# The half-filled last products of v and u moved behind the scores and put side by side in the row halves of the TensorE array

## The chip, the core and the metric

The kernel runs on one core of a Trainium2 chip. Its time is the device time of one execution in microseconds (us). Of the kernel before, three runs took 307.78, 306.66 and 303.63 us, a median of 306.66. A fourth execution was recorded by the hardware profiler and took 303.61 us.

## The reference: what is computed

Three blocks follow each other, for 2 batches of 768 tokens, all in 32-bit floats.

1. A gated recurrent attention (mLSTM) of 8 heads of 40 features. Per step t: C = f C + i v k^T, n = f n + i k, y = sigmoid(o) * (C q) / max(|n q|, 1), with stabilised gates. Its output x has 8 * 40 = 320 features per token.
2. A gated MLP: h = relu(x @ w_in), w_in of 320 x 1024; u is the first half of the 1024 columns, v the second. v is normalised over its 512 columns, mixed over the tokens with w_spatial (768 x 768), a bias is added, the result is multiplied by u and by w_out.
3. A second MLP with a token shift: k = relu(xk @ w_k), out = sigmoid(xr @ w_r) * (k*k @ w_v).

The change touches x @ w_in of block 2 alone.

## The kernel before

**Tiling.** The 1536 tokens are 12 chunks of 128 (NU = 12). The attention works by chunk, in its chunked form: scores of the 128 queries against the 128 keys, values, a carried state between chunks. Products that want more precision than the one-pass type float32r are made of parts: a tensor is split in hi (rounded) and lo (the rest), and hi*hi + hi*lo + lo*hi is summed in PSUM.

**x @ w_in.** x has 320 features, so its feature-major copy is three tiles of 128, 128 and 64 rows: TA, TB and TL ("left"). The TL tile has its 64 features twice, in the rows 0 to 63 and 64 to 127 of the array; xth holds the hi parts and xtl the lo parts, each twice. Tile 4 of win holds the hi part of the last 64 rows of w_in in the rows 0 to 63 and their lo part in the rows 64 to 127. `parts` (L1265) so makes eight products: three for TA, three for TB, and two for TL. The first TL product (win tile 4 by xth) gives hi*hi + lo*hi, all 128 rows put to use. The second (win tile 4 by xtl) gives hi*lo, which is wanted, and lo*lo, which isn't: it is the half-filled product. `v_product(u)` (L1376) has x as the stationary operand and moves 512 columns of w_in, into bank ps_v, for one chunk. `u_product(g, m)` (L1400) has 128 columns of w_in as the stationary operand and moves 384 tokens (three chunks, a block g) of x, into bank ps_e. Both call `chain` (L1251), whose matmul is L1254.

**Order of the work.** All of it is written out by hand, an engine's program each, tied by semaphores. TensorE's runs over slots u = 2 to 13. A slot holds, in this order: `state(u-1)` (L1358, bank ps_z), `values(u-1, 1)` (L1339, ps_in), `carry(u-1)` (L1349, ps_out), `scores(u)` (L1329, ps_s0 and ps_s1), `v_product(u-2)`, in slots 3 and 4 `spread_decay(u)` (L1294), up to slot 4 `factors_to_tokens(u+1)` (L1283), `values(u, 0)`, one `u_product`, `x_transposed(u-1)` (L1368, ps_t), and in slots 7, 10 and 13 a second `u_product`. The u products lie in slots 4 to 13 (`u_tiles`), as x of a block of three chunks must be there. Scores are 64-row products: heads of the one group lie in the rows 0 to 63 of the array, of the other in 64 to 127, and the two alternate, into two banks.

**The other engines.** ScalarE reads ps_v (L644) and ps_e (`u_relu`, L661), rounds x (L655) and the parts of w_in (`win_left_hi`, L681 and L682), and takes the exponentials (L637). The hi of the last 64 rows that is subtracted for lo lies for a while in a free place of vnh (`win_left`). VectorE multiplies scores by exponentials (L946), makes x from values and gates (L980 to L1008, `outputs`), takes lo of x (L1026) and of w_in (`win_lo_of`, L1050), adds the state (L972), copies decays (L938) and normalises v. GpSimd and the DMA queues play no part in the change. After slot 13 TensorE runs the groups of blocks 2 and 3, one after the other (all L1254), with the eight banks in turn.

Of the kernel before, what the change touches and what calls it, by code (L numbers as in the profile page):

```python
# [27 lines left out]
ACT = mybir.ActivationFunctionType  # L28

B, H, S, D = 2, 8, 768, 40  # L30
DM, DF = H * D, 1024
HF = DF // 2
CH = 128
NC = S // CH
NU = B * NC
# [6 lines left out]
NB = 384  # L42
NBLK = B * S // NB
UPB = NB // CH
# [3 lines left out]
TA, TB, TL = 0, 1, 2  # L48
# [35 lines left out]
def u_tiles(slot):  # L84

    out = []
    for g in range(NU // UPB):
        first = UPB * g + UPB + 1
        for m, s in enumerate((first, first + 1, first + 2, first + 3)):
            if s == slot and g < NU // UPB - 1:  # L90
                out.append((g, m))
    return out
# [3 lines left out]
U_AT = {x: n for n, x in enumerate(U_ORDER)}  # L96
# [98 lines left out]
def program(nc, qk, vk, og, fg, ig, w_in, w_sp, b_sp, mu, w_out, w_k, w_v, w_r, out):  # L195
# [14 lines left out]
    win = at("win", [128, 5, DF], WIN, F32R)  # L210
    win_raw = at("win_raw", [128, 3, DF], WIN + 8192)
    ut = at("ut", [128, B, 4, S], UT)
    vnh = [at(f"vnh{b}", [128, NC, HF], VN + b * 24576, F32R) for b in range(B)]
# [10 lines left out]
    xtl = at("xtl", [128, 2, 3, NB], XT + 9216, F32R)  # L224
# [96 lines left out]
    with ExitStack() as ctx:  # L321
        names = ["ps_s0", "ps_s1", "ps_e", "ps_in", "ps_out", "ps_z", "ps_t", "ps_v"]
        ps_s0, ps_s1, ps_e, ps_in, ps_out, ps_z, ps_t, ps_v = [
            ctx.enter_context(nc.psum_tensor(n, [128, 512], F32)) for n in names]
# [15 lines left out]
        sems = {}  # L340
# [12 lines left out]
        def win_left(n):  # L353

            if n == 0:
                return vnh[0][64:128, NC - 2, :]
            return vnh[0][64:128, NC - 1, 128 * (n - 1):128 * n]

        def bits(ap):

            return ap.bitcast(F32)
# [232 lines left out]
        def _(act):  # L594
            sc = nc.scalar
# [82 lines left out]
            def win_left_hi(n):  # L678
                c = WIN_PART[n]
                act.wait_ge(sems[f"win_in{min(n, 1)}"], 64)  # L680
                sc.activation(win_left(n), win_raw[64:128, 2, c], ACT.Copy).then_inc(sems["win_left"], 1)  # L681
                sc.activation(win[0:64, 4, c], win_raw[0:64, 2, c], ACT.Copy).then_inc(sems["win_hi"], 1)  # L682

            def win_rows_hi(n):
                c = WIN_PART[n]
# [122 lines left out]
            for p, key in enumerate(GROUPS):  # L808
# [36 lines left out]
                if kind == "k":  # L845
                    n = 8 * a + b
# [28 lines left out]
        def _(dve):  # L875
            ve = nc.vector
# [170 lines left out]
            def win_lo_of(n):  # L1047
                c = WIN_PART[n]
                dve.wait_ge(sems["win_left"], n + 1)
                ve.tensor_tensor(win[64:128, 4, c], win_raw[64:128, 2, c], bits(win_left(n)),  # L1050
                                 ALU.subtract).then_inc(sems["win_left_lo"], 1)
                dve.wait_ge(sems["win_hi"], 3 * n + 3)
                ve.tensor_tensor(win[:, 2, c], win_raw[:, 0, c], bits(win[:, 0, c]),
                                 ALU.subtract).then_inc(sems["win_lo"], 1)
# [122 lines left out]
            for p, key in enumerate(GROUPS):  # L1177
                kind, a, b = key
                ps = bank_of[p % 8]
                if kind == "sp":  # L1180
                    n = 4 * a + b
# [41 lines left out]
                if kind == "k":  # L1223
                    n = 8 * a + b
# [12 lines left out]
                if kind == "v":  # L1237
                    n = UPB * a + b
# [9 lines left out]
        def _(pe):  # L1248
            te = nc.tensor

            def chain(dst, pairs):  # L1251

                for n, (w, x) in enumerate(pairs):
                    last = te.matmul(dst, w, x, start=n == 0, stop=n == len(pairs) - 1)  # L1254
                return last

            def parts(w, x):

                out = []
                for t in (TA, TB):
                    out += [(w(0, t), x(0, t)), (w(0, t), x(1, t)), (w(1, t), x(0, t))]
                return out + [(w(0, TL), x(0, TL)), (w(1, TL), x(1, TL))]  # L1265

            def split_rows(w, cols):

                def tile(part, t):
                    return w[:, 4 if t == TL else t + 2 * part, cols]  # L1270
                return tile
# [99 lines left out]
            def x_tiles(g, cols):  # L1371
                def tile(part, t):
                    return (xth, xtl)[part][:, g % 2, t, cols]
                return tile

            def v_product(u):  # L1376
                pe.wait_ge(sems["xt_hi_done"], u + 1)
                pe.wait_ge(sems["xt_lo_done"], u + 1)
                if u == 0:

                    pe.wait_ge(sems["win_hi"], 3)
                    pe.wait_ge(sems["win_left_lo"], 1)
                    pe.wait_ge(sems["win_lo"], 1)
                    pe.wait_ge(sems["win_lo_pool"], 1)
                if u == 0:
                    pe.wait_ge(sems["exp_done"], 2 * EARLY)
                pe.wait_ge(sems["v_read"], u)
                x = x_tiles(u // UPB, slice((u % UPB) * CH, (u % UPB + 1) * CH))
                chain(ps_v[:, :], [(x_, w_) for w_, x_ in parts(split_rows(win, slice(HF, DF)), x)]
                      ).then_inc(sems["v_mm"], 1)  # L1390

            def u_chain(dst, g, m):
                if g == 0:
                    pe.wait_ge(sems["win_hi"], 3 * (m + 2))
                    pe.wait_ge(sems["win_left_lo"], m + 2)
                    pe.wait_ge(sems["win_lo"], m + 2)
                    pe.wait_ge(sems["win_lo_pool"], m + 2)
                return chain(dst, parts(split_rows(win, slice(m * 128, m * 128 + 128)), x_tiles(g, slice(0, NB))))

            def u_product(g, m):  # L1400
                pe.wait_ge(sems["gwt_done"], 5)
                pe.wait_ge(sems["u_read"], U_AT[g, m])
                u_chain(ps_e[:, 0:NB], g, m).then_inc(sems["u_mm"], 1)


            pe.wait_ge(sems["vr_zero"], 1)
# [18 lines left out]
            for u in range(2, NU + 2):  # L1425
                if u == 2:
                    spread_decay(2)
                if u <= NU:
                    if chunk(u - 1) < NC - 1:
                        state(u - 1)  # L1430
                    if u == 4:
                        x_transposed(2)
                    values(u - 1, 1)
                    if chunk(u - 1) > 0:
                        carry(u - 1)
                    if u in (2, 3):
                        x_transposed(u - 2)
                if u < NU:
                    scores(u)
                if u == NU + 1:  # L1440

                    u_product(*u_tiles(u)[0])
                v_product(u - 2)
                if 3 <= u < NC - 1:
                    spread_decay(u)
                if u < NC - 1:
                    factors_to_tokens(u + 1)
                if u < NU:
                    values(u, 0)
                if u_tiles(u) and u <= NU:  # L1450
                    u_product(*u_tiles(u)[0])
                if 4 <= u <= NU:
                    x_transposed(u - 1)
                for g, m in u_tiles(u)[1:]:
                    u_product(g, m)
# [3 lines left out]
            for p, key in enumerate(GROUPS):  # L1459
# [4 lines left out]
                if kind == "u":  # L1464
                    last = u_chain(ps[:, 0:NB], a, b)
                elif kind == "sp":
# [12 lines left out]
                    pairs = []  # L1479
# [111 lines left out]
```

## Time and profile before

| what | us |
|---|---|
| three runs | 307.78, 306.66, 303.63 |
| the profiled execution's own time | 303.61 |
| its span, first to last instruction | 301.9 |
| TensorE matmuls busy in it | 291.7 (97%) |
| VectorE busy | 203.1 (67%) |
| ScalarE busy | 160.6 (53%) |
| GpSimd busy | 65.0 (22%) |
| mean granted clock of TensorE | 0.983 of full |

The own time is 1.7 us above the span. In the rows below PE is TensorE, PEld its weight loads, DVE VectorE, ACT ScalarE. A matmul of 32-bit floats is two records, one of float32r is one. Matmuls are pipelined, so a record's length is mostly latency, and what a product costs is read from start to start.

### The profile page before, as it was taken

How to read it: one execution, taken by the hardware profiler on the slowest of the kernel's cores; microseconds unless marked ns; L12 is line 12 of the kernel's file. 1: busy time of each engine (PE TensorE's matmuls, PEld its weight loads, DVE VectorE, ACT ScalarE, POOL GpSimd, SP SyncE). 2: the span in 40 equal slices, each digit the busy share in tenths (PEclk: the TensorE clock that was granted, in tenths of full speed). 3: DMA queues.
4: the chain of work that ended last, by engine and by line, in shares of the span. 5: the costliest groups of instructions: out<-in, count | busy, mean ns of one | idle time of the engine just before them, and what ended most of it. 6: DMA issues, size and time to landing. Idle time of an engine off the chain costs nothing.

```text
span 301.9 us, 5393 instructions
## 1 busy us (share of the span) xinstructions
PE 291.7 (97%) x1904; PEld 278.6 (92%) x1904; DVE 203.1 (67%) x434; ACT 160.6 (53%) x365; POOL 65.0 (22%) x93
## 2 busy tenths in 40 slices
PE   7999898999999999999999999998999999999996
PEld 3898787998999898999999999997999999999995
DVE  6899889898788588446416888768764276655111
ACT  5747675793456456331136567598672467255000
POOL 6143345343344332612101203200000000000000
PEclk9977979999999999999999999999999999999999
DMA  4779951473472162000060020500001000100111
GB/s 133 229 212 280 334 163 66 157 213 105 138 245 85 21 244 88 0 2 0 14 196 0 0 67 1 175 2 0 0 2 43 22 2 2 46 22 0 43 46 43
DMA packets 12922, 25.99 MB, mean 86 GB/s; under 512 B 2016, under 2 KB 5696, under 8 KB 12896
## 3 DMA queue, kind: packets, MB, share of 16 engines
q1 hardware_dynamic: 12720, 25.12, 27.2%
q10 hardware_dynamic: 176, 0.53, 0.4%
q8 instruction: 15, 0.25, 0.3%
q14 instruction: 11, 0.09, 0.1%
HBM read 23.63 MB, written 2.02 MB: 85 GB/s over the span
## 4 chain that ended last, share of the span: by engine, by line
PE 88%; DVE 5%; ACT 3%; DMA 2%; issue 1%; SPq 0%; ACTq 0%; DVEq 0%
PE ps_v L1254 15%; PE ps_e L1254 13%; PE ps_s L1254 12%; PE ps_out L1254 7%; PE ps_in L1254 7%; PE ps_t L1254 7%; PE ps_in L1339 6%; PE ps_z L1254 6%; PE ps_s L1329 5%; PE ps_out L1349 3%; DMA wv_raw<-in_w_v 2%; PE ps_z L1358 2%; PE ps_v L1408 2%; PE ps_t L1368 1%; DVE pt L946 1%
## 5 line engine op out<-in xcount | busy, mean ns | idle before, releaser
L1339 PEld LDWEIGHTS ps_in<-tok,pt 128*128 128x128 f32 x192 | 24.6, 197 | 2.0 <-DVE pt L946 1.3
L1226 DVE TENSOR_TENSOR kr<-kr 128x384 f32<-128x384 f32 x32 | 17.7, 558 | 12.5 <-ACT kr L850 12.5
L1339 PE MATMUL ps_in<-tok,pt 128*128 128x42 f32 x192 | 25.1, 282 | 0.7 <-DVE pt L946 0.7
L637 ACT ACTIVATE et<-mb,gwt 128x128 f32<-128x128 f32 x80 | 24.7, 392 | 1.0 <-POOL mb L546 0.9
L822 ACT ACTIVATE gh<-ut 128x384 fp32r<-128x384 f32 x16 | 8.4, 525 | 30.2 <-DVE ut L1192 30.2
L1254 PE MATMUL ps_v<-win,xth 128*128 128x512 f32 x60 | 21.5, 423 | 0.1
L585 POOL TENSOR_TENSOR gl<-ut,gh 128x384 fp32r<-128x384 f32 x8 | 9.0, 1122 | 53.1 <-ACT gh L822 53.1
L1254 PE MATMUL ps_e<-xth,win 128*128 128x384 f32 x60 | 17.3, 353 | 0.9 <-ACT ut L661 0.9
L1174 DVE TENSOR_TENSOR kkl<-kr,kkh 128x384 fp32r<-128x384 f32 x32 | 17.7, 553 | 0.7
L946 DVE TENSOR_TENSOR pt<-ps_s,et 128x512 f32<-128x512 f32 x24 | 16.5, 688 | 1.4 <-PE ps_s L1329 0.7
L806 ACT ACTIVATE kkh<-kr 128x384 fp32r<-128x384 f32 x32 | 16.7, 522 | 1.3 <-DVE kr L1226 1.3
L1165 DVE SCALAR_TENSOR_TENSOR shifted<-yt,omm,scaled 128x384 f32<-128x384 f32 x24 | 15.3, 641 | 2.6 <-ACT scaled L801 2.0
L539 POOL TENSOR_SCALAR rstd<-mv 128x1 f32<-128x1 f32 x12 | 6.1, 508 | 45.8 <-DVE mv L1014 45.8
L1329 PE MATMUL ps_s<-qkt 64*128 64x128 f32 x192 | 15.8, 310 | 0.0
L648 ACT ACTIVATE vnh<-vnf 128x512 fp32r<-128x512 f32 x12 | 7.6, 634 | 14.4 <-DVE vnf L1019 14.3
L1254 PEld LDWEIGHTS ps_v<-win,xth 128*128 128x128 f32 x60 | 11.6, 194 | 3.8 <-issue 0.7
L801 ACT ACTIVATE scaled<-yt,mucol 128x384 f32<-128x384 f32 x24 | 14.6, 606 | 0.1
L1329 PEld LDWEIGHTS ps_s<-qkt 64*128 64x128 f32 x192 | 13.3, 210 | 1.3 <-issue 0.7
L1254 PE MATMUL ps_v<-win,xtl 128*128 128x512 f32 x36 | 14.3, 398 | 0.0
L661 ACT ACTIVATE ut<-ps_e 128x384 f32<-128x384 f32 x12 | 5.9, 490 | 13.1 <-PE ps_e L1254 13.1
L1254 PEld LDWEIGHTS ps_e<-xth,win 128*128 128x128 f32 x60 | 11.0, 188 | 1.7 <-issue 1.6
L1349 PE MATMUL ps_out<-zt,qkt 128*128 128x84 f32 x80 | 12.2, 301 | 0.0
(325 smaller groups left out, 883.1 us busy)
## 6 DMA issues: line engine op xcount, KB each, us to landing
mb<-maxima SPq DMA_DIRECT2D x9, 512.0 KB, 5.8
tok<-in_vk SPq DMA_DIRECT2D x12, 328.0 KB, 4.3
qkt<-in_qk SPq DMA_DIRECT2D x24, 160.0 KB
sp_raw<-in_w_sp SPq DMA_DIRECT2D x6, 384.0 KB, 5.0
out_y<-ob SPq DMA_DIRECT2D x12, 160.0 KB, 1.8
wv_raw<-in_w_v SPq DMA_DIRECT2D x2, 640.0 KB, 5.3
win_raw<-in_w_in SPq DMA_DIRECT2D x4, 256.0 KB, 6.1
wk_raw<-in_w_k SPq DMA_DIRECT2D x2, 512.0 KB, 4.7
```

Source lines behind the costliest of these rows:

```text
L585: gp.tensor_tensor(g[1][:, b, :], ut[:, a // 2, b, (a % 2) * NB:(a % 2) * NB + NB], bits(g[0][:, b, :]), ALU.subtract).then_inc(sems["g_lo ...
L637: last = sc.activation(et[:, j, h, :], mb[u % 2][:, HH * j + h, :], ACT.Exp, bias=gwt[:, chunk(u), x:x + 1], scale=-1.0)
L801: sc.activation(scaled[:, n % 2, :], yt[a % 2][:, t, 1:NB + 1], ACT.Copy, scale=mucol[:, w, t:t + 1]).then_inc(sems["x_scaled"], 1)
L806: sc.activation(kkh[(n // 8) % 2][:, n % 8, :], kr[n % 4][:, :], ACT.Copy).then_inc(sems["kk_hi_done"], 1)
L946: ve.tensor_tensor(pt[:, j, :, :], ps_s[j][:, :].rearrange("p (h t) -> p h t", h=HH), et[:, j, :, :], ALU.mult).then_inc(sems["probs_done" ...
L1165: ve.scalar_tensor_tensor(shifted[:, n % 2, :], y[:, t, 0:NB], omm[:, w, t:t + 1], scaled[:, n % 2, :], ALU.mult, ALU.add).then_inc(sems[" ...
L1174: ve.tensor_tensor(kkl[(n // 8) % 2][:, n % 8, :], kr[n % 4][:, :], bits(kkh[(n // 8) % 2][:, n % 8, :]), ALU.subtract).then_inc(sems["kk_ ...
L1226: ve.tensor_tensor(kr[n % 4][:, :], kr[n % 4][:, :], kr[n % 4][:, :], ALU.mult).then_inc(sems["kk_done"], 1)
L1254: last = te.matmul(dst, w, x, start=n == 0, stop=n == len(pairs) - 1)
L1329: last = te.matmul(ps_s[r][:, g * CH:(g + 1) * CH], keys[u % NS][rows, g, :], queries[u % NS][rows, g, :], start=True, stop=True)
L1339: last = te.matmul(p_in[:, HH * j + h, :], pt[:, j, h, :], vt[u % 2][:, HH * j + h, :], start=True, stop=True)
L1349: last = te.matmul(p_out.rearrange("p (r g) d -> p r g d", r=2)[:, :, g, :], queries[u % NS][:, g, :], zt[(u - 1) % 2][:, g, :, :], start= ...
```

## The change

Tile 4 of win is swapped for the v columns (part 0): hi now lies in the rows 64 to 127 and lo in 0 to 63; the u columns stay as they were. In the slots 4 to 11 a new `left_products` is issued right behind `scores(u)`: it makes only hi*lo of the last 64 features, for v in the array's rows 64 to 127 into ps_v, and for the slot's first u product in the rows 0 to 63 into ps_e. These two open the accumulation in their banks. In the same slots `v_product` and the first `u_product` go on in the open bank, with seven products each and no longer the eighth. The slots 2, 3, 12 and 13, the second u products of the slots 7 and 10, and the u products that follow the slots are as before.

```diff
         def win_left(n):
             if n == 0:
-                return vnh[0][64:128, NC - 2, :]
+                return vnh[0][0:64, NC - 2, :]
             return vnh[0][64:128, NC - 1, 128 * (n - 1):128 * n]
+        def left_rows(n):
+            return (slice(0, 64), slice(64, 128)) if n == 0 else (slice(64, 128), slice(0, 64))
...
-                sc.activation(win_left(n), win_raw[64:128, 2, c], ACT.Copy).then_inc(sems["win_left"], 1)
-                sc.activation(win[0:64, 4, c], win_raw[0:64, 2, c], ACT.Copy).then_inc(sems["win_hi"], 1)
+                lo, hi = left_rows(n)
+                sc.activation(win_left(n), win_raw[lo, 2, c], ACT.Copy).then_inc(sems["win_left"], 1)
+                sc.activation(win[hi, 4, c], win_raw[hi, 2, c], ACT.Copy).then_inc(sems["win_hi"], 1)
...
-                ve.tensor_tensor(win[64:128, 4, c], win_raw[64:128, 2, c], bits(win_left(n)),
+                lo, _ = left_rows(n)
+                ve.tensor_tensor(win[lo, 4, c], win_raw[lo, 2, c], bits(win_left(n)),
...
-            def chain(dst, pairs):
+            def chain(dst, pairs, opened=False):
-                    last = te.matmul(dst, w, x, start=n == 0, stop=n == len(pairs) - 1)
+                    last = te.matmul(dst, w, x, start=n == 0 and not opened, stop=n == len(pairs) - 1)
-            def parts(w, x):
+            def parts(w, x, opened=False):
-                return out + [(w(0, TL), x(0, TL)), (w(1, TL), x(1, TL))]
+                return out + [(w(0, TL), x(0, TL))] + ([] if opened else [(w(1, TL), x(1, TL))])
...
+            def left_products(u, g, m):
+                pe.wait_ge(sems["xt_hi_done"], u + 1)
+                pe.wait_ge(sems["xt_lo_done"], u + 1)
+                pe.wait_ge(sems["v_read"], u)
+                pe.wait_ge(sems["win_hi"], 3 * (m + 1) + 1 if g == 0 else 15)
+                pe.wait_ge(sems["gwt_done"], 5)
+                pe.wait_ge(sems["u_read"], U_AT[g, m])
+                t = slice((u % UPB) * CH, (u % UPB + 1) * CH)
+                te.matmul(ps_v[:, :], xtl[64:128, (u // UPB) % 2, TL, t], win[64:128, 4, HF:DF], start=True, stop=False)
+                te.matmul(ps_e[:, 0:NB], win[0:64, 4, m * 128:m * 128 + 128], xtl[0:64, g % 2, TL, :],
+                          start=True, stop=False)
...
-                v_product(u - 2)
+                opened = u < NU and len(u_tiles(u)) > 0
+                if opened:
+                    left_products(u - 2, *u_tiles(u)[0])
+                v_product(u - 2, opened)
...
                 if u_tiles(u) and u <= NU:
-                    u_product(*u_tiles(u)[0])
+                    u_product(*u_tiles(u)[0], opened)
```

## Rows read from the trace of the kernel before

**Rows 1.** The page's busy shares, and the busy time of three stretches (clock before DMA).
```profile
PE 291.7 (97%) x1904; PEld 278.6 (92%) x1904; DVE 203.1 (67%) x434; ACT 160.6 (53%) x365; POOL 65.0 (22%) x93
...
49.00:111.00 62.00, 61.31 (x487) 56.72 (x485) 51.09 (x127) 37.09 (x98) 25.84 (x36) 1.00 0.45 141
119.90:205.00 85.10, 85.10 (x494) 85.10 (x493) 53.97 (x93) 44.53 (x88) 16.93 (x16) 1.00 0.14 41
207.20:298.90 91.70, 91.70 (x584) 91.62 (x584) 46.89 (x91) 40.50 (x88) 0.00 (x0) 1.00 0.06 21
```
**Rows 2.** TensorE's waits, 49 to 111 us (the slots 5 to 11): total, times, longest.
```profile
PE ps_e L1254 <- ACT ut L661: 0.7, 2, 0.3
```
**Rows 3.** TensorE's timeline in slot 9: start, length, engine, line, operation, count.
```profile
85.12 1.16 PE L1329 MATMUL ps_s<-qkt 64*128 64x128 f32 x16
86.21 0.50 PE L1254 MATMUL ps_v<-win,xth 128*128 128x512 f32 x1
86.55 0.39 PE L1254 MATMUL ps_v<-win,xtl 128*128 128x512 f32 x1
...
88.17 0.98 PE L1339 MATMUL ps_in<-tok,pt 128*128 128x42 f32 x8
88.98 0.42 PE L1254 MATMUL ps_e<-xth,win 128*128 128x384 f32 x1
89.24 0.34 PE L1254 MATMUL ps_e<-xtl,win 128*128 128x384 f32 x1
...
90.47 0.49 PE L1368 MATMUL ps_t<-ident,xg 128*128 128x128 f32 x3
90.80 0.88 PE L1358 MATMUL ps_z<-tok,kw 128*104 128x84 f32 x8
```
**Rows 4.** The last two records of the scores, in flight at 86.19 us; all scores of slots 5 to 11.
```profile
86.00 0.28 PE L1329 MATMUL ps_s<-qkt 64*128 64x128 f32 x2
...
L1329 PE MATMUL ps_s<-qkt x112: 272/272/373, 51.6 to 104.5; 64*128 64x128 f32 x112
```
**Rows 5.** TensorE's timeline in slot 4, and the granted clock (0.50) from 39.64 us.
```profile
40.40 2.08 PE L1329 MATMUL ps_s<-qkt 64*128 64x128 f32 x16
42.41 0.78 PE L1254 MATMUL ps_v<-win,xth 128*128 128x512 f32 x1
...
44.66 0.29 PE L1294 MATMUL ps_z<-gwt,ident 128*128 128x16 f32 x2
...
48.60 0.55 PE L1368 MATMUL ps_t<-ident,xg 128*128 128x128 f32 x3 [1.21 <-DVE xg L1008]
39.64:43.04 3.40, 3.40 (x23) 0.50 0.25 72
```
**Rows 6.** VectorE's timeline in slot 4.
```profile
44.99 0.17 DVE L938 COPY dec<-ps_z 128x16 f32<-128x16 f32 x1 [1.30 <-PE ps_z L1294]
```
**Rows 7.** Before slot 7's and slot 8's v product: lo of x on VectorE; u_relu on ScalarE.
```profile
65.56 0.55 DVE L1026 TENSOR_TENSOR xtl<-ps_t,xth 128x384 fp32r<-128x384 f32 x1
...
67.53 0.50 PE L1254 MATMUL ps_v<-win,xth 128*128 128x512 f32 x1
...
74.45 0.49 ACT L661 ACTIVATE ut<-ps_e 128x384 f32<-128x384 f32 x1 [1.45 <-PE ps_e L1254]
...
77.93 0.50 PE L1254 MATMUL ps_v<-win,xth 128*128 128x512 f32 x1
```
**Rows 8.** Slot 7: the last step of x on VectorE, and what follows on TensorE.
```profile
71.56 0.20 DVE L1008 COPY xg<-xg 128x64 f32<-128x64 f32 x1
...
71.93 0.49 PE L1368 MATMUL ps_t<-ident,xg 128*128 128x128 f32 x3
72.77 0.41 PE L1254 MATMUL ps_e<-xth,win 128*128 128x384 f32 x1 [0.34 <-ACT ut L661]
```
**Rows 9.** The last step of x on VectorE in slot 9; VectorE's waits, 49 to 111 us.
```profile
89.71 0.20 DVE L1008 COPY xg<-xg 128x64 f32<-128x64 f32 x1
...
DVE inter L980 <- PE ps_out L1349: 4.2, 5, 1.1
```

More of the change, by code:

```diff
@@ L1374, in x_tiles, with v_product @@
                 return tile
-            def v_product(u):
+            def v_product(u, opened=False):
                 pe.wait_ge(sems["xt_hi_done"], u + 1)
@@ L1388, in v_product, with u_chain @@
                 x = x_tiles(u // UPB, slice((u % UPB) * CH, (u % UPB + 1) * CH))
-                chain(ps_v[:, :], [(x_, w_) for w_, x_ in parts(split_rows(win, slice(HF, DF)), x)]
-                      ).then_inc(sems["v_mm"], 1)
-            def u_chain(dst, g, m):
+                chain(ps_v[:, :], [(x_, w_) for w_, x_ in parts(split_rows(win, slice(HF, DF)), x, opened)],
+                      opened).then_inc(sems["v_mm"], 1)
+            def left_products(u, g, m):
[9 more added lines that the diff above has]
+                          start=True, stop=False)
+            def u_chain(dst, g, m, opened=False):
                 if g == 0:
@@ L1397, in u_chain, with u_product @@
                     pe.wait_ge(sems["win_lo_pool"], m + 2)
-                return chain(dst, parts(split_rows(win, slice(m * 128, m * 128 + 128)), x_tiles(g, slice(0, NB))))
-            def u_product(g, m):
+                return chain(dst, parts(split_rows(win, slice(m * 128, m * 128 + 128)), x_tiles(g, slice(0, NB)), opened),
+                             opened)
+            def u_product(g, m, opened=False):
                 pe.wait_ge(sems["gwt_done"], 5)
                 pe.wait_ge(sems["u_read"], U_AT[g, m])
-                u_chain(ps_e[:, 0:NB], g, m).then_inc(sems["u_mm"], 1)
+                u_chain(ps_e[:, 0:NB], g, m, opened).then_inc(sems["u_mm"], 1)
             pe.wait_ge(sems["vr_zero"], 1)
```

## The prediction

> **What bounds the kernel now.** I read the page's busy shares first, then the busy time by stretch, then TensorE's waits, and last its timeline slot by slot. TensorE is busy for 97% of the span, and in the stretches that matter it is more than that: from 49 to 111 us, the slots 5 to 11, it lacks 0.7 of 62 us, and in the two long stretches of the MLP groups it lacks nothing [rows 1]. In the slots 5 to 11 its only wait is that of the second u products of the slots 7 and 10 for their bank, 0.7 us in all [rows 2]. So what TensorE is spared in these slots comes off the end, as long as nothing else is late within the same slot. Slot 4 is the exception: its transposes start 1.21 us late, for VectorE's x [rows 5].
>
> **What is taken away.** In each of eight slots one v product of 512 columns and one u product of 384. Their cost is the distance from start to start, not the record's length. In slot 9 the second v product starts at 86.55 and the next work at 88.17: seven products in 1.62 us, 0.23 each. The second u product starts at 89.24 and the transposes at 90.47: seven in 1.23, 0.18 each [rows 3]. The first product of either chain costs more (0.34 and 0.26), but it stays the first. Taken away per slot: 0.23 + 0.18 = 0.41 us.
>
> **What is added.** Two products of 64 rows, one in each row half, 512 and 384 columns. The trace shows no float32r product in a row half, but it shows the scores. In slot 9 their last two records start together, at 86.00, and both are over 0.28 us later, when a single one takes 0.272 [rows 4]. Sixteen records take 1.09 us (85.12 to 86.21), 0.07 each, where full-height transposes with as many columns take 0.11 each (three in 90.47 to 90.80) [rows 3]. So the two halves do run side by side, a pair per 0.11 us. If the new pair does so too, it costs what its longer member costs, 0.23 us. The change of the array from halves to full height is paid now as well: the first v product starts at 86.21, 0.21 us behind the last pair [rows 3, 4], where the next pair would have come after 0.11; the other 0.10 is the change. It is paid once, before and after, as the new pair stands in the same mode as the scores. **Bounds:** from below 0.13, if the pair's stream hid that 0.10; from above, one behind the other, 0.41; and further up, one behind the other at the pace of a 32-bit record of the scores (0.11 us for 128 columns, 0.87 ns a column), 0.45 + 0.34 = 0.79 us. I take 0.23, because the scores are the nearest rows: the same row halves, two banks, straight before. Per slot 0.41 - 0.23 = 0.18 us is saved.
>
> The Trainium skill has a rule that speaks for less: its page "TensorE: Matmul & The Clock Gate", section "Measured speedup vs the span model", gives 3.07 times for four products of 32 rows and 512 columns, not four times. By that shortfall, an estimate, the pair would cost 0.23 * 4 / 3.07 = 0.30 us and a slot would save 0.11. Rows 4 show no such loss for the scores.
>
> **Slot 4.** Here the u product's saving goes into the wait that is there anyway: the transposes wait for VectorE's x, and the chain to it starts with the decays (L938) at 44.99, which wait for the small product at 44.66 behind v [rows 5, 6]. What counts in this slot is thus when v ends. In the profiled execution the granted clock is 0.50 from 39.64 to 43.04 and the scores of this slot take 2.01 us instead of 1.09, 1.84 times as long [rows 3, 5]. The new pair stands at 42.3 in that stretch: 0.23 * 1.84 = 0.43. The v product that is gone stood behind 43.04, at 0.23. So v ends 0.20 later, and so do the decays, x and the slot. In an execution where the clock is full here, it is 0.0.
>
> **The waits that are added** stand in front of v, where v's own already stood: x of the chunk, and ps_v read. Lo of x is there at 66.11 in slot 7 for a v at 67.53, 1.4 us ahead [rows 7], and that is the least of the eight slots. New are the bank of u and its weights. The bank was read last by u_relu of the slot before; the tightest place is slot 8, where u_relu ends at 74.94 and v starts behind the scores at 77.93, 3 us later [rows 7]. In slot 11 it stands alike. The hi part of w_in is made a slot ahead. All this costs nothing. If such a wait did bite, v, the values and the u product would be queued behind it, and VectorE's probabilities would not be, since the scores are already out. The swapped halves of tile 4 are the same number of instructions over as many rows on ScalarE and VectorE: nothing. No DMA is moved, and no queue of SyncE or GpSimd is passed.
>
> **What is late next.** The transposes in each slot now come 0.18 earlier against VectorE's chain. In slot 9 x is ready at 89.91 for a start at 90.47, 0.56 ahead [rows 3, 9], enough. In slot 7 it is ready at 71.76 for 71.93: 0.11 of the 0.18 fits [rows 8] and some 0.06 is lost before the transposes. But behind them the second u product waits for u_relu until 72.77, and that goes by the end of the first u product, so nothing of it reaches the slot's end. The savings of earlier slots move VectorE along with TensorE: it waits for the carried product in five of the slots, 4.2 us in all [rows 9], and has slack to follow. Behind the slots TensorE has no idle time that could swallow anything in the stretches shown [rows 1].
>
> **The sum.** Seven slots at 0.176 (0.231 + 0.176 - 0.231) are 1.23 us off, slot 4 gives 0.20 back: 1.0 us off. The profiled execution, 303.61 us with 301.9 of span and 1.7 around it, becomes 302.6. The runs of before spread over 4 us: two executions at 303.6, two at 306.7 and 307.8, with a mean of the four of 305.4 and a median of the three of 306.66. Less 1.0 these are 304.4 and 305.7. A median of the changed kernel is as likely by the one as by the other, so I say **305.0 us**, which is 1.0 below a base of 306.0.
>
> **The rivals**, on the same base of 306.0 us.
> *Side by side, but not wholly:* the pair costs between 0.23 and 0.41, with the middle, 0.32, as its mark. Then a slot saves 0.09, seven save 0.6, and slot 4 gives back 0.32 * 1.84 - 0.23 = 0.36: 0.3 off, 305.7. For it speaks that the members are of unequal length, which the scores' are not; against it, rows 4. Chance 0.12. By the page's estimate, 0.30, it would be 0.11 a slot, 0.8, less 0.3 in slot 4: 305.5.
> *The change doesn't do what it says:* the halves run one behind the other, at 0.41. The seven slots give nothing, and slot 4 loses 0.41 * 1.84 - 0.23 = 0.5 us: 306.5. For it: nothing shown of float32r in halves. Against it: the scores use the same two row halves and two banks [rows 4]. Chance 0.10.
> *Slower, one mechanism:* a half-height float32r product streams like a record of the scores, at 0.87 ns a column. Its place is the pair in each slot. Side by side it costs 0.45, 0.04 more than was saved: 0.3 for seven slots, and 0.45 * 1.84 - 0.23 = 0.6 in slot 4, 0.9 slower, 306.9. Behind each other it costs 0.79: 7 * 0.38 and 0.79 * 1.84 - 0.23 = 1.2 in slot 4, 3.9 slower, 309.9. It decides from a pair of 0.41 us on. For it: 0.11 us for 128 columns in the scores; against: that is equally the time of a weight load, as the full-height values of 42 columns start no closer (eight in 88.17 to 88.98) [rows 3]. Chance 0.06 and 0.02.
>
> **How the numbers follow.** The forecast, 1.0 off, has 0.70; the rivals have 0.12, 0.10 and 0.08. The range is mostly the spread of the runs: its low end is the fast executions less the full saving with slot 4 at full clock, 303.6 - 1.4 = 302.2; its high end is the slow ones, 307.3 as a mean, less 0.1, which takes in the first two rivals: 307.2. About 2 in 10 are left out. What a measurement of this kernel tells from no change is about 2%, 6.1 us. To be faster by that, each of eight slots would have to save 0.77 us, more than the two products cost together: 0.01. To be slower by it the pair would have to cost 1.2 us: 0.02. Within 2%: 0.97.
>
> **What would show it.** In the timeline of slot 9 two float32r records of 64 rows should start within 0.01 us of each other, 0.11 behind the last scores; the first full v product should start some 0.44 us behind the last scores, not 0.21; scores to the end of v should stay as long as before, and the u chain should be 0.18 shorter. The scores of the slots 5 to 11, from 51.6 to 104.5 [rows 4], should stand 1.1 us closer together. Two 64-row records with starts 0.2 us apart would show the second rival, a first v product 0.65 behind the scores the third. A wait of TensorE for ut or xtl in front of the pair would prove me wrong on the waits, and a wait for xg in more slots than 4 and 7 would prove me wrong on VectorE's slack.

## The result, and the profile after

The changed kernel took 304.08 us, the median of 20 runs from 299.32 to 308.18, beside 306.19 for the kernel before (20 runs, 302.80 to 309.20). The ratio is 0.990, 95% interval [0.985, 0.994]: 1% faster, within the 2% that counts as the same. In a second series the same kernel came out at 305.39 (12 runs) beside 305.00 (35 runs), ratio 1.008 [1.003, 1.012]. (A ratio leaves out, of either kernel, the executions more than 1.5% above its own fastest, so it can differ from the ratio of the medians, which is 0.993 in the first series and 1.001 in the second.) The two intervals exclude each other, so one ratio alone is not to be trusted here; what the change is worth has to be read from the trace.

The profiled execution took 302.88 us with a span of 301.2. The page's shares and the two long MLP stretches are as before, TensorE without a gap in them [rows 1]; the columns are TensorE, weight loads, VectorE, ScalarE, GpSimd, then clock and DMA:

```profile
PE 290.9 (97%) x1904; PEld 276.5 (92%) x1904; DVE 202.4 (67%) x434; ACT 160.5 (53%) x365; POOL 64.0 (21%) x93
...
49.40:110.50 61.10, 60.34 (x488) 54.98 (x486) 50.93 (x127) 37.04 (x98) 25.53 (x36) 1.00 0.45 143
119.38:204.48 85.10, 85.10 (x494) 85.10 (x493) 53.95 (x93) 44.72 (x88) 16.93 (x16) 1.00 0.13 41
206.70:298.20 91.50, 91.50 (x584) 91.40 (x583) 46.66 (x91) 40.30 (x88) 0.00 (x0) 1.00 0.06 21
```

TensorE's timeline of slot 9 of the changed kernel answers to [rows 3]:

```profile
85.10 1.16 PE L1336 MATMUL ps_s<-qkt 64*128 64x128 f32 x16
86.01 0.42 PE L1409 MATMUL ps_e<-xtl,win 64*128 64x384 f32 x1
86.02 0.48 PE L1408 MATMUL ps_v<-win,xtl 64*128 64x512 f32 x1
86.43 0.50 PE L1261 MATMUL ps_v<-win,xth 128*128 128x512 f32 x1
...
88.16 0.98 PE L1346 MATMUL ps_in<-tok,pt 128*128 128x42 f32 x8
88.97 0.42 PE L1261 MATMUL ps_e<-xth,win 128*128 128x384 f32 x1
...
90.28 0.49 PE L1375 MATMUL ps_t<-ident,xg 128*128 128x128 f32 x3
```

The two new products (L1409 and L1408) start within 0.01 us of each other. From the scores' start to the values it takes 3.06 us, where it took 3.05 before (85.12 to 88.17): the pair costs what v's last product cost. From the u product's start to the transposes it takes 1.31 instead of 1.49: the 0.18 of the u product is gone.

The lengths of the slots, from the first record of the scores to the next slot's (slot 11: to v behind it), read from the traces of the profiled executions, before, after and of the experiments that follow. From slot 5 on, after and again, the one kernel that was profiled twice, agree to 0.01 us; and where two kernels do the same work in a slot other than 7, they agree to 0.02 us, in executions from 299 to 306 us. So the slots tell hundredths where the clocked times don't tell a microsecond:

```
kernel        slot 3   slot 4   slot 5  6     7      8     9     10     11    sum 5 to 11
before          9.02    11.18    7.52  7.34  10.40  8.28  8.27  10.25  7.38   59.44
after           8.69    11.49    7.35  7.17  10.44  8.10  8.10  10.09  7.20   58.45
again          10.23    10.92    7.35  7.17  10.44  8.10  8.10  10.09  7.20   58.45
same_half       9.58    12.37    7.52  7.34  10.27  8.28  8.28  10.27  7.38   59.34
from_slot5     10.06    10.91    7.35  7.17  10.44  8.09  8.10  10.09  7.20   58.44
lo_early       11.27    11.33    7.35  7.32  11.35  8.09  8.10  10.09  7.21   59.51
lo_prev        10.17    11.09    7.35  7.17  10.10  8.10  8.10  10.09  7.20   58.11
short_mask      9.55    11.28    7.34  7.17  10.09  8.11  8.10  10.09  7.20   58.10
v_alone         9.66    12.12    7.53  7.35  10.38  8.27  8.28  10.27  7.39   59.47
den_early       7.93     8.39    7.34  7.17  10.10  8.09  8.10  10.09  7.20   58.09
den_before      7.92     8.55    7.52  7.34  10.26  8.27  8.28  10.25  7.38   59.30
```

Six of the seven slots from 5 on are 0.16 to 0.18 us shorter after the change. Slot 7 is not: it is 0.04 longer.

### The profile page after: what moved, and what is told of

It is laid out like the page before. It is cut to its first block, busy times and chain, and to the rows that moved or that the text cites. A ratio compares the mean times of both kernels' runs of the same rounds, so it can differ in the third digit from the quotient of the medians.

```text
span 301.2 us, 5417 instructions
## 1 busy us (share of the span) xinstructions
PE 290.9 (97%) x1904; PEld 276.5 (92%) x1904; DVE 202.4 (67%) x434; ACT 160.5 (53%) x365; POOL 64.0 (21%) x93
## 4 chain that ended last, share of the span: by engine, by line
PE 90%; DVE 5%; ACT 3%; issue 1%; DVEq 0%; ACTq 0%
PE ps_v L1261 15%; PE ps_s L1261 13%; PE ps_e L1261 13%; PE ps_out L1261 7%; PE ps_t L1261 7%; PE ps_in L1261 7%; PE ps_z L1261 7%; PE ps_in L1346 6%; PE ps_s L1336 5%; PE ps_out L1356 3%; PE ps_z L1365 2%; PE ps_v L1429 2%; PE ps_t L1375 1%; DVE pt L952 1%; DVE den L997 1%
## 5 line engine op out<-in xcount | busy, mean ns | idle before, releaser
L795 ACT ACTIVATE xr<-shifted 128x384 fp32r<-128x384 f32 x12 | 6.3, 522 | 10.9 <-DVE shifted L1172 10.9
```

## The experiments

**again: the changed kernel once more.** No edit.

> The changed kernel once more. Theory A (the profile's sum): it is 0.7 to 1.1 us faster than the kernel before, ratio 0.9965, and what the first comparison showed beyond that (about 1%, 3 us) is the scatter of the granted clock between executions. Theory B: the change saves some 3 us, of which the two profiled executions show only a part; then the ratio is again at 0.99 or below. In the profile the pair's two records start 0.006 us apart and scores to the end of v take 3.05 us as before.

Measured: slots 5 to 11 as after, to 0.01 us; median 305.39, ratio 1.008 [1.003, 1.012]. Theory B is out. The slots bear out theory A, but its ratio of 0.9965 lies outside the interval as well: a ratio of these series is not good to half a per cent. Up to slot 5 the executions differ: slot 3 takes 8.69 us in after and 10.23 in again, slot 4 11.49 and 10.92, with where the stretches of granted clock 0.5 fall and how long they are. In this execution they go from 20.0 to 26.8 and from 40.5 to 43.9; in the others each is 3.4 or 6.8 us long, or the first is absent. Over the kernel before, the changed one and three of its variants (same_half, from_slot5, lo_early), the execution time goes with the mean granted clock, 2.1 us for each 0.01. With that slope taken out, 32 executions of the changed kernel stand 0.9 us below the 63 of the kernel before whose clock was recorded, with a standard error of 0.27. So the gain is 0.4 to 1.4 us (95%), and the traces' 1.0 in the slots 5 to 11 lies in it.

**same_half: both products in the same row half.**

```diff
-            return vnh[0][64:128, NC - 1, 128 * (n - 1):128 * n]
+            return vnh[0][0:64, NC - 1, 128 * (n - 1):128 * n]
-            return (slice(0, 64), slice(64, 128)) if n == 0 else (slice(64, 128), slice(0, 64))
+            return slice(0, 64), slice(64, 128)
...
-                te.matmul(ps_e[:, 0:NB], win[0:64, 4, m * 128:m * 128 + 128], xtl[0:64, g % 2, TL, :],
+                te.matmul(ps_e[:, 0:NB], win[64:128, 4, m * 128:m * 128 + 128], xtl[64:128, g % 2, TL, :],
```

> Changed kernel, but all parts of win's tile 4 are swapped and both new products lie in the rows 64 to 127: same instructions, same place, same waits, only not in different halves. Theory side by side: they now run one behind the other, the pair costs 0.41 us instead of 0.23 (0.60 us from the first to the first full v product instead of 0.41), 0.18 more in each of slots 5, 6, 8 to 11, so 1.1 to 1.3 us slower than the changed kernel. Rival (a half-height product is cheap by itself, or it is only the place behind the scores that helps): no difference to the changed kernel.

TensorE's timeline of slot 9 in same_half:

```profile
87.46 0.48 PE L1408 MATMUL ps_v<-win,xtl 64*128 64x512 f32 x1
87.78 0.33 PE L1409 MATMUL ps_e<-xtl,win 64*128 64x384 f32 x1
88.04 0.50 PE L1261 MATMUL ps_v<-win,xth 128*128 128x512 f32 x1
```

Now the u product starts 0.32 us behind the v product, and the first full product 0.58 behind, where it was 0.41. Slots 5, 6 and 8 to 11 are as long as in the kernel before, to 0.02 us, and together 1.06 us longer than in after; slot 7, at 10.27, is shorter than in both (see lo_prev). The saving is all from lying side by side; a half-height product by itself is not cheaper, and the place behind the scores gives nothing. The times (305.26 median, ratio 1.005 [1.000, 1.010]) agree but would not have shown it.

**v_alone: only v in its half.** The u product of `left_products` is left out and `u_product` has its eighth product back.

> Changed kernel with only the v product in its row half behind the scores; the u product is full height and has its eighth product back. Theory side by side: the half-height v product costs what the full one cost, 0.23, so the slots 5, 6, 8 to 11 are as long as in the kernel before (7.52, 7.34, 8.28, 8.27, 10.25, 7.38), and all of the 0.18 us per slot is the u product that hides beside it. Rival (half-height products are cheaper, or the place behind the scores is): slots shorter than before.

Measured: slots as in the kernel before, to 0.02 us. One execution, 305.65 us. The v product in its half costs the 0.23 us of the full one, and the u product beside it is free.

**from_slot5: slot 4 without the pair.**

```diff
-                opened = u < NU and len(u_tiles(u)) > 0
+                opened = 4 < u < NU and len(u_tiles(u)) > 0
```

> Changed kernel, with the pair in the slots 5 to 11 alone; slot 4 is as in the kernel before. Theory: in slot 4 nothing can be gained, since the transposes wait for VectorE's x, and the pair delays v and the decays, by 0.3 us in the profile after; without it slot 4 (scores to scores) is 0.2 to 0.3 us shorter where the granted clock is half there, and the kernel 0.2 to 0.3 faster. Rival (slot 4 was longer only because the half clock fell elsewhere): slot 4 as long as in the changed kernel.

Measured: slot 4 takes 10.91 us, beside 10.92 in again and 11.49 in after. The rival is right: slot 4 was longer because more of the half clock fell in it. Against the decays' small product (L1301 after, L1294 before) it splits cleanly. Behind it, up to the scores of slot 5, there are 6.92 us in before, after, again and from_slot5 alike (to 0.01), with and without the pair: the u product's saving is swallowed by the wait for x, 1.37 us after the change where it was 1.21 [rows 5]:

```profile
49.06 0.33 PE L1375 MATMUL ps_t<-ident,xg 128*128 128x128 f32 x1 [1.37 <-DVE xg L1014]
```

Ahead of it there are 4.26 us before (40.40 to 44.66) and 4.57 after (40.55 to 45.12). The half clock ended at 43.04 and 43.88. Time at half clock counted by half, that is 2.94 and 2.91 us at full clock: no more work after than before. Two later profiles show it without such counting: in den_before and den_early the clock is full here, and this part takes 3.05 us without the pair and 3.06 with it. The median of 304.21 (ratio 1.002 [0.997, 1.007]) doesn't tell it from the others.

**lo_early: lo of w_in ahead of the probabilities.** In slot 7 the changed kernel has a new wait on TensorE, in front of the u product (the label "issue" stands for a wait whose releaser the profile doesn't name):

```profile
69.62 0.98 PE L1346 MATMUL ps_in<-tok,pt 128*128 128x42 f32 x8
70.78 0.41 PE L1261 MATMUL ps_e<-xth,win 128*128 128x384 f32 x1 [0.18 <-issue]
```

VectorE of that slot, and GpSimd's decay of the state (L538) and mask (L551), in the changed kernel:

```profile
68.36 1.53 DVE L1025 TENSOR_SCALAR vnf<-vr,mv,rstd 128x512 f32<-128x512 f32 x1
69.92 0.29 DVE L1057 TENSOR_TENSOR win<-win_raw,vnh 64x128 fp32r<-64x128 f32 x1
70.24 0.29 DVE L1060 TENSOR_TENSOR win<-win_raw,win 128x128 fp32r<-128x128 f32 x1
...
67.79 0.76 POOL L538 TENSOR_TENSOR zdec<-zt,dec 104x336 f32<-104x336 f32 x1
68.51 1.10 POOL L551 TENSOR_SCALAR_AFFINE_SELECT mb<-mb 128x1024 f32<-128x1024 f32 x1
```

The lo parts of w_in for this u product (L1057, L1060) are ready at 70.53. They stand behind vnf (the normalised v), which takes 1.53 us where it takes 0.54 in most slots, and which ends just behind the mask's end at 69.61. The edit:

```diff
+                if u > 4 and u - 1 in WIN_AT:
+                    win_lo_of(WIN_AT[u - 1])
                 if u < NU:
                     probabilities(u, 0)
...
-                if u > 4 and u - 1 in WIN_AT:
-                    win_lo_of(WIN_AT[u - 1])
```

> Changed kernel, with VectorE's lo of w_in (win_lo_of) put ahead of the first probabilities in slots 5 to 7, instead of behind the normalising of v. Theory: slot 7 saved nothing because its u product waits for this lo (values to u product 1.16 us instead of 0.81), which stands behind a vnf that GpSimd's mask holds up for 1 us; now the u product starts on time, slot 7 is 0.2 to 0.35 us shorter (10.1 to 10.2 instead of 10.45), the kernel 0.2 to 0.3 faster. Rival: x of the slot (VectorE's last copy) is late anyway and holds the transposes, so that slot 7 stays as long, at most 0.1 shorter.

Measured: slot 7 takes 11.35 us, 0.91 longer; median 305.91, ratio 1.010 [1.005, 1.015]. Both theory and rival were wrong about the edit. VectorE and GpSimd in lo_early:

```profile
70.23 0.39 DVE L1057 TENSOR_TENSOR win<-win_raw,vnh 64x128 fp32r<-64x128 f32 x1
70.65 1.79 DVE L1060 TENSOR_TENSOR win<-win_raw,win 128x128 fp32r<-128x128 f32 x1
72.36 0.68 DVE L952 TENSOR_TENSOR pt<-ps_s,et 128x512 f32<-128x512 f32 x1
...
70.43 0.82 POOL L538 TENSOR_TENSOR zdec<-zt,dec 104x336 f32<-104x336 f32 x1
71.20 1.10 POOL L551 TENSOR_SCALAR_AFFINE_SELECT mb<-mb 128x1024 f32<-128x1024 f32 x1
```

Now it is the lo operation that is held until the mask ends at 72.30, and the probabilities, which all of TensorE waits for, stand behind it (1.01 us of wait). In the plain order the probabilities had slipped in ahead.

**lo_prev: the same lo at the end of the slot before.** Only part 4, at the end of VectorE's slot 6:

```diff
-                if u > 4 and u - 1 in WIN_AT:
+                if 4 < u < 7:
                     win_lo_of(WIN_AT[u - 1])
...
                     if u <= NU:
                         x_low(u - 1)
+                    if u == 6:
+                        win_lo_of(WIN_AT[6])
```

> Changed kernel; only the lo of w_in that slot 7's u product needs (win_lo_of of part 4) is moved, to the end of VectorE's slot 6, behind lo of x. Theory (slot 7 saves nothing because this lo stands behind a vnf that GpSimd's mask holds up): the u product of slot 7 starts 0.81 us behind the values instead of 1.16, vnf is held up as before but holds nobody, slot 7 takes 10.1 to 10.2 us instead of 10.44; slots 5, 6, 8 to 11 as in the changed kernel. Rival (VectorE is simply full in slots 5 to 7): the 0.6 us put in front of the state only shifts the delay to values or transposes, slot 6 or 7 lose what is won.

TensorE's timeline of slot 7 in lo_prev:

```profile
72.03 0.98 PE L1348 MATMUL ps_in<-tok,pt 128*128 128x42 f32 x8
72.83 0.42 PE L1263 MATMUL ps_e<-xth,win 128*128 128x384 f32 x1
```

Values to u product 0.80 us, slot 7 10.10 instead of 10.44, slot 6 unchanged at 7.17. The theory holds. In the kernel before, slot 7 had a piece of this wait too (values at 69.50, u product at 70.45 in its timeline, 0.95 apart), and same_half, whose slot 7 is 10.27 and whose vnf there takes 0.54 us, shows that its size goes with small shifts between VectorE and GpSimd. One execution, 305.06 us.

**short_mask: is it GpSimd that holds VectorE?** The mask covers one of the eight heads:

```diff
-                gp.affine_select(out=mb[u % 2][:, :, :], in_=mb[u % 2][:, :, :], compare_op=ALU.is_ge, fill=-NEVER,
-                                 base=0, pattern=[[0, H], [1, CH]],
+                gp.affine_select(out=mb[u % 2][:, 0:1, :], in_=mb[u % 2][:, 0:1, :], compare_op=ALU.is_ge, fill=-NEVER,
+                                 base=0, pattern=[[0, 1], [1, CH]],
```

> Changed kernel; GpSimd's mask of the maxima covers one head of eight (an eighth of the elements; the output is then not the reference's), all else as it is. Theory (the mask and the state's decay on GpSimd hold up VectorE): vnf in slot 7 takes 0.54 us instead of 1.53 and slot 7 10.1 instead of 10.44; in slot 4 the den operation takes below 1.2 instead of 1.81 and from the decays to the next scores it takes below 6.4 us instead of 6.92. Rival (these are waits for semaphores that the trace puts into the operation): durations stay at 1.53 and 1.81.

The den operation of slot 4 in the changed kernel, and GpSimd beside it:

```profile
45.73 1.81 DVE L997 SCALAR_TENSOR_TENSOR den<-num 128x8 f32<-128x8 f32 x1
...
45.71 0.76 POOL L538 TENSOR_TENSOR zdec<-zt,dec 104x336 f32<-104x336 f32 x1 [4.10 <-DVE dec L944]
46.42 1.10 POOL L551 TENSOR_SCALAR_AFFINE_SELECT mb<-mb 128x1024 f32<-128x1024 f32 x1
```

VectorE in short_mask, slot 4 and slot 7:

```profile
46.54 0.76 DVE L997 SCALAR_TENSOR_TENSOR den<-num 128x8 f32<-128x8 f32 x1
...
68.22 0.67 DVE L1025 TENSOR_SCALAR vnf<-vr,mv,rstd 128x512 f32<-128x512 f32 x1
...
68.92 0.29 DVE L1057 TENSOR_TENSOR win<-win_raw,vnh 64x128 fp32r<-64x128 f32 x1
```

The den operation falls from 1.81 us to 0.76, vnf from 1.53 to 0.67 (I had said 0.54; 0.13 of the state's decay on GpSimd is left), and slot 7 to 10.09. From the decays to the scores of slot 5 it takes 5.98 us (45.93 to 51.91) instead of 6.92. So the long VectorE operations are GpSimd's doing. One execution, 302.18 us. The Trainium skill says so in a rule of its page "SBUF — State Buffer", section "Summary: rules for kernel authors": when VectorE is in a mode that uses both ports or has two SBUF inputs, and the GpSimd operation reads SBUF, the second to issue blocks until the first is done. The trace agrees as far as this goes: all three long operations start while GpSimd's decay of the state is running (68.36 within 67.79 to 68.55, 45.73 within 45.71 to 46.47, and in lo_early 70.65 within 70.43 to 71.25). But they are held longer than by the decay: the mask, recorded as starting 0.15 to 0.69 us behind them, is done first too. They end at 69.89, 47.54 and 72.44, the mask at 69.61, 47.52 and 72.30. With the short mask the den operation ends at 47.30, just behind the decay (47.27) and ahead of the short mask (47.86). So an operation can be held by more than one of GpSimd's in a row; why the short mask doesn't hold it is left open.

**den_early: outputs ahead of the decays.** VectorE stands still in front of the decays of slot 4 (1.30 us [rows 6], 1.65 after the change), while the values that x is made from have been there since 42.7 (both after the change). With lo_prev, and:

```diff
+                if u in (3, 4):
+                    outputs(u - 1)
                 if u < NC - 1:
                     decays(u)
                     factors_by_token(u + 1)
...
-                if u <= NU:
+                if 4 < u <= NU:
                     outputs(u - 1)
```

> A version meant to beat both: the changed kernel with lo_prev, and in VectorE's slots 3 and 4 the outputs (den to x) go ahead of the decays and factors, for which VectorE waits 1.65 us in slot 4. Theory: x is ready before TensorE asks for it, the transposes of slot 4 start 1.2 to 1.4 us earlier, the u product's saving counts there too, and from the decays to the scores of slot 5 it takes 5.4 to 5.6 us instead of 6.92; slot 3 gains up to 0.9. With slot 7 the kernel is 1.5 to 2.7 us faster than the changed kernel at the same granted clock. Rival: the decays, now behind five operations, come late for the state or the next factors, or what is saved in the slots 3 and 4 is lost again to a half-clock stretch; then 0.5 us or less.

TensorE's and VectorE's timeline of slot 4 in den_early:

```profile
41.02 1.16 PE L1340 MATMUL ps_s<-qkt 64*128 64x128 f32 x16
...
44.09 0.29 PE L1305 MATMUL ps_z<-gwt,ident 128*128 128x16 f32 x2
...
46.49 0.49 PE L1379 MATMUL ps_t<-ident,xg 128*128 128x128 f32 x3
...
49.41 0.38 PE L1340 MATMUL ps_s<-qkt 64*128 64x128 f32 x2
...
43.98 0.17 DVE L997 SCALAR_TENSOR_TENSOR den<-num 128x8 f32<-128x8 f32 x1
...
45.57 0.20 DVE L1014 COPY xg<-xg 128x64 f32<-128x64 f32 x1
45.68 0.17 DVE L944 COPY dec<-ps_z 128x16 f32<-128x16 f32 x1
```

The den operation takes 0.17 us, as it no longer meets GpSimd's decay and mask, which wait for the decays themselves. x is ready at 45.77, ahead of the transposes, and from the decays' product to the scores of slot 5 it takes 5.32 us instead of 6.92. Slot 4 takes 8.39, slot 3 7.93. The time was 298.51 (6 runs, 297.35 to 299.79) beside 305.97 (11 runs), ratio 0.976 [0.972, 0.981]. That is 7.5 us between the medians, against the kernel before. What I expected, 1.5 to 2.7, was against the changed kernel and at the same clock. Counted at full clock as above, slot 3 is 0.72 us shorter than in after, slot 4 1.43 and slot 7 0.34: 2.5 us, within it. Between the means of the executions, 304.5 and 298.6, it is 5.9 us. A little is given back in the slots, as the rival had it: TensorE now waits once for the decays, 0.5 us (total, times, longest):

```profile
PE ps_z L1369 <- DVE dec L944: 0.5, 1, 0.5
```

The rest goes with the clock: the mean granted clock of its executions is 0.992, beside 0.982 for the changed kernel. In this profile nothing falls to half from 28.5 us to the end of the work:

```profile
28.60:298.00 269.40, 264.17 (x1756) 1.00 0.23 75
```

**den_before and den_early2: the pair where nothing else waits.** den_before is the kernel before with the same two moves on VectorE, den_early2 is den_early again.

> The kernel before (no pair in row halves), with the two moves on VectorE of den_early. Theory: where TensorE has no wait left in slots 4 and 7, each of the eight slots is longer by 0.18 us than in den_early: slot 4 8.57 instead of 8.39, slot 7 10.28 instead of 10.10, slots 5 to 11 together 59.3 instead of 58.1, and the kernel is 1.4 us slower than den_early (some 300 us, against 298.5), still 6 us faster than the kernel before. Rival (the two moves only work as the pair has freed VectorE or TensorE): no gain against the kernel before beyond 2 us.

> den_early once more, on the same chip and in the same rounds as den_before, for their difference. Theory: 1.4 us faster than den_before (8 slots of 0.18), with a scatter of the executions small enough to show it, since there are fewer half-clock stretches to fall in. Rival: 0.7 us, as the plain kernels differ, or nothing.

Measured: den_before slot 4 8.55, slot 7 10.26, slots 5 to 11 59.30, all as expected to 0.02 us. Its median is 300.31 (12 runs, 299.33 to 300.79), ratio to the kernel before 0.991 [0.987, 0.996]; den_early2's is 299.30 (6 runs), 0.988 [0.981, 0.994]. In these same rounds the pair is worth 1.2 us (means of 300.2 and 299.0), plus or minus 0.6, which alone doesn't exclude the rival's 0.7. With the first six executions, which are from another chip, it is clearer: both sets of den_early have a mean of 298.8 (12 runs, standard deviation 0.7), den_before 300.2 (0.6): the pair is worth 1.4 us, plus or minus 0.5 (95%), which is 8 times 0.18, and the slots 4 to 11 of the traces give 1.37. The kernel before has a standard deviation of 2.2 over its 63 runs. The better version than both is den_early: 298.8 beside 305.0 for the kernel before, in means over all executions, 6.2 us or 2.0%; the ratios of its two series, 0.976 and 0.988, leave open whether it is more than 2%. Of the 6.2 the VectorE moves bring 4.8 and the pair 1.4.

How much of the 4.8 is the clock can be told in two ways. Slots 3, 4 and 7 of den_before, counted at full clock, are 0.7, 1.3 and 0.1 us shorter than before: 2.2. And some executions had full clock all through (a mean of 0.999 or 1.000): 6 of the kernel before with a mean of 300.6, 2 of the changed kernel at 299.7, 2 of den_before at 299.3 and one of den_early at 297.4. By these the moves are worth 1.3 us, the pair 0.9 to 2.0, from very few executions. So 1.3 to 2.2 of the 4.8 are waits that are gone, and over half goes with the clock.

## Why the prediction was right, and where not

**The size.** I said 305.0 us in 302.2 to 307.2 and the median was 304.08. I said 1.0 us less; the traces give 1.0 in the slots 5 to 11 (59.44 to 58.45), the times at equal clock 0.9. (The 307.3 at the range's high end is 307.2 from the two executions that it is the mean of.) But two terms of my sum were wrong and cancelled. That the total came out right is in part luck: I had 1.23 off in seven slots and 0.20 back in slot 4, the traces have 0.99 and 0.0. Nor do the times test it: the range held my base of 306.0, no gain at all, as well.

**The cost of the pair, right.** 0.23 us for both, read off the scores as the nearest rows. From the scores' start to the values nothing changed (3.05 and 3.06), the first full product stands 0.41 behind the pair's start, and same_half shows 0.58 when they don't overlap. From the last scores to the first full product it is 0.44, as I said, but I had it made up otherwise: the pair follows the scores by 0.03, not 0.11, and the 0.08 comes back behind it. The rivals "not wholly side by side" and "one behind the other" are ruled out. The 3.07 of 4 that I took from the Trainium skill's page "TensorE: Matmul & The Clock Gate", section "Measured speedup vs the span model", doesn't hold for this pair either: by that a slot would have saved 0.11, it saved 0.17. The slower rival, a half-height product at 0.87 ns a column, is out by v_alone: 512 columns cost 0.23.

**Slot 4, mis-sized.** I charged 0.20 us because the pair ran at half clock while the product it replaced had run at full. That is wrong as a way of counting. The stretch at half clock has its own length; what is put into it pushes other work out of it into full clock. The one that reaches into slot 4 was 3.41 us long in before, after, again, from_slot5 and lo_prev, with whatever stood in it. Counted in full-clock time the part of slot 4 up to the decays is 2.94 before and 2.91 after. The term should be 0.0, and the u product's saving there is indeed lost in the wait for x, as I had said.

**Slot 7, the failed step.** I let the first 0.06 be lost in front of the transposes and said that "nothing of it reaches the slot's end". Slot 7 saved nothing at all. I had looked at x and at the bank's reader, and not at the third thing that the u product of a first block waits for, the lo part of its weights on VectorE. It was already 0.14 late before (values to u product 0.95 us, not the 0.81 of slot 9 [rows 3]), which I could have read. And VectorE did not move along with TensorE, as my step "what is late next" had it: in slots 5 and 6 it is nearly full. The busy time of those two slots in the kernel before, the stretch ahead, then its length, TensorE, weight loads, VectorE:

```profile
51.58:59.10 7.52, 7.52 (x60) 6.92 (x60) 6.65 (x18) 4.64 (x15) 2.56 (x5) 1.00 0.47 158
59.10:66.44 7.34, 7.34 (x60) 6.78 (x59) 6.95 (x19) 6.73 (x18) 3.12 (x6) 1.00 0.62 176
```

TensorE's scores of slot 7 come 0.12 us later than before (66.44 and 66.56), but what stands on GpSimd comes 0.34 later. Here are vnf and the mask before the change:

```profile
68.24 1.31 DVE L1019 TENSOR_SCALAR vnf<-vr,mv,rstd 128x512 f32<-128x512 f32 x1
...
68.17 1.10 POOL L546 TENSOR_SCALAR_AFFINE_SELECT mb<-mb 128x1024 f32<-128x1024 f32 x1
```

The mask starts at 68.51 instead of 68.17, vnf ends at 69.89 instead of 69.55, and the u product starts at 70.78 instead of 70.45. Against the scores that is 0.21 later; the missing product gives 0.18 back, and the slot is 0.04 longer. lo_prev and short_mask each remove the hold by another way, and either gives 0.34 us. For the same reason the scores of the slots 5 to 11 stand 0.81 us closer together, not the 1.1 that I had as a sign.

**The added waits, right.** No record of TensorE waits in front of the pair in any slot. Nor does it wait for x in the slots 5 to 11.

## What to carry to other kernels

Two half-height products next to work that already runs in row halves cost only the longer of them (that is where it was measured here): look for the half-filled last pieces of a 320-row contraction and pair them there. Before spending effort on 0.2 us pieces of a full engine, look at each wait that is left on it, and ask whether the engine it waits for was itself standing still: here one wait of 1.2 us on TensorE was VectorE waiting, out of order, for TensorE, and undoing it, with its like in slot 3, gave three times what the pair gave, more than half of it through the clock. And where executions scatter by 2 us, compare slots of the trace, which agree to 0.02 where the work is the same.

## What the runs showed of the hardware

**Where slot 3's wait for x is gone, the clock didn't fall.** In nine profiled executions (all but those of den_early and den_before) TensorE waits 0.7 to 1.9 us for x in slot 3, up to a point between 37.2 and 40.4 us. The granted clock then goes to half, 1.2 GHz, 0.4 to 2.5 us later, from a point between 38.8 and 42.4 us on, for 3.4 or 6.8 us. The kernel before:

```profile
37.51 0.55 PE L1368 MATMUL ps_t<-ident,xg 128*128 128x128 f32 x3 [0.86 <-DVE xg L1008]
```

Its clock fell at 39.6. In the three executions of den_early and den_before, where TensorE is not kept waiting there for x, the clock stayed at 2.4 GHz from 28.5 us at the latest to 296.8 at the earliest. That is seen in twelve executions, not tried wait by wait, and it is no rule for every wait: the wait of slot 4, 1.2 to 1.4 us in eight of the nine, has no fall behind it in any, and the executions of the kernel before with full clock all through show that the fall can stay out. But it goes with how much was won: between the profiles of the kernel before and den_before slot 4 is 2.6 us shorter and slot 3 1.1, where the waits themselves were 1.2 and 0.9, and the mean of the executions fell by 4.8.

**Row halves go their own way.** The program issues v's product ahead of u's. In the trace of the changed kernel u's record (rows 0 to 63) starts 0.006 us ahead of v's (rows 64 to 127), in each of the slots. The likely reason is in the scores ahead of it, which alternate between the halves 0.007 us apart: in slot 9 their last two records start at 85.983 and 85.990, and each of the two new products starts 0.03 us behind the last score of its own half, at 86.014 and 86.020. In same_half, with one half for both, the order is the program's.

**A small VectorE operation can take 1.8 us.** The den operation on 128 x 8 elements took 1.81 us beside GpSimd's decay and mask, 0.76 with a short mask and 0.17 without either beside it; a lo of 128 x 128 took 1.79 us instead of 0.29.
